# Attention and two MoE layers on one core: where the weight sums of the second layer are made, a second PSUM bank for h, and row moves between ring loads

## The chip, the cores and the metric

The kernel runs on one core of one Trainium2 chip. The metric is the device time of the whole program in microseconds. The kernel before takes 974.08 us (median of three runs, 971.9 to 975.14).

## What is computed

The reference, cut to what matters:

```
def phi(x):                                   # x: (4, 8, 576, 64), omega: (128, 64)
    h = einsum('bhsd,md->bhsm', x, omega) - sum(x * x, -1) / 2
    return exp(h - max(h, -1)) / sqrt(128)
q_p, k_p = phi(q * scale), phi(k * scale)
kv, z = einsum('bhsm,bhsd->bhmd', k_p, v), sum(k_p, axis=2)
attn = (q_p @ kv) / (q_p @ z + 1e-6)          # 4 batches, 8 heads, 576 tokens, 64 wide
x = attn, heads side by side                  # 2304 tokens x 512
h = x @ w_in;   x = (h * clip(h + 3, 0, 6) / 6) @ w_out          # layer 1: 512 -> 2048 -> 512
h = x @ w_in2;  out = (h * sigmoid(1.702 * h)) @ w_out2          # layer 2, same sizes
```

## The kernel before

Every fp32 product is made of three fp32r products of a high part (a rounded copy) and a low part (the value less the copy): high x high, high x low, low x high.

Heads are worked in 16 pairs. Pairs 0 to 4 come first. Pairs 5 to 15 lie inside layer 1. Layer 1 takes the 2304 tokens in chunks of 512, 512, 512, 512 and 256 columns, and each chunk in J = 16 steps n (80 steps). TensorE makes in step n the 12 matmuls of `hidden(n)` into the one PSUM bank `hid`, then the 12 of `output(n - 1)` (6 of 512 columns in the last chunk). Between the two come a unit of an attention pair and behind the second another: each step has two slots g = 2n and 2n + 1, a pair has 8 slots, and its units are in `UNITS` ("q", "tail"; "cross"; "k"; "moves"; none; "kv" with the feature parts; "nd0"; "nd1"). So a new pair begins every fourth step. `hidden(n)` waits on `gated`, until VectorE has read h of step n - 1 out of the bank.

ScalarE makes of h the factor R (`gate`), VectorE multiplies (`gated_block`), ScalarE rounds the product (`high`) and VectorE takes the low part (`low`). In the attention units ScalarE also makes exps, high features (`q_hi`), half of the block moves of q (`moves`, DMAs on its own queue) and the quotient's parts; VectorE makes maxima, biases, the transposes `cross`, the states and low features. GpSimd squares and folds rows of q and k (`square_rows`), which VectorE sums (`norms`) for the biases: the squares of q of pair a + 2 at slot 7 of pair a, those of k of pair a + 1 at slot 2.

Layer 2 is computed by a scheme with 7 products of quarter matrices for 8, for tokens in three parts of 768. It needs sums of quarters of its weights. They are made in 32 half-units u on the way (`load_raw`, `prepare`, `high_combos`, `store_combos`): SP loads 128 x 512 raw weights, GpSimd makes four sums of 128 x 128, ScalarE rounds raw (128 x 384) and sums (128 x 512), GpSimd takes the two low parts, SP stores four pieces (high and low of 384 and 512 columns) to the DRAM tensor `combos`. Of the 32 half-units the first EARLY_PREP = 10 are at every second step from step 14, in one buffer (a free part of X); the others are at steps 49 to 63 and then at every second, in three buffers `stage`. Each engine works through its own list in order, and a wait holds all that stands behind it; SP's list holds, in this order around an early half-unit: the block moves of q (behind `cross`), the stores of half-unit u, the load of u + 1 (which waits until those stores have landed), the columns of the next pair, the stores of u + 1, the load of u + 2, the rows of q, the values and the rows of k.

In layer 2 TensorE takes a unit of 12 matmuls of 384 columns for every 512 KB block that SP loads from `combos` into a ring of 10 slots (`load_combos`). The ring's first 10 loads are put between layer 1's last steps. The last chunk of layer 1 comes out by rows; VectorE transposes it in 32 x 32 blocks (`turned_rows`), and 32 DMAs of 16 KB move the blocks to their places in X (`row_move`). They are needed for the last third of layer 2.

## Time and profile before

| | before |
|---|---|
| median of 3 runs | 974.08 us |
| the profiled execution, its own time | 973.57 us |
| its span | 971.8 us |
| busy: PE, DVE, ACT, POOL | 892.7, 552.6, 428.6, 433.8 us |
| 134 + 34 ring loads, KB each, us to landing | 512.0 KB, 4.4 and 4.3 us |

The span is 1.8 us less than the profiled execution's own time, and that is 0.5 us under the median. PE's busy time has modelled ends, so a stretch of 100% is not a full one; its idle time and the granted clock are the more useful columns. Slots and steps stand in the trace in order: the "q" unit of a pair is the first group of L908 on PE, nd0 is L988.

### The profile page before, as it was taken

The numbers are of one execution on the slowest core, as the hardware profiler recorded it, in microseconds if no ns is written. First come the engines' busy times: TensorE is split into PE (matmuls) and PEld (weight loads), VectorE is DVE, ScalarE is ACT, GpSimd is POOL, SyncE is SP. The second block draws the span as 40 slices with busy tenths as digits, with TensorE's granted clock in tenths as the row PEclk, the third lists the DMA queues.
The fourth block names the chain that finished last, engine by engine and source line by source line (L and its number), as shares of the span: only waits on it lengthen the run. The fifth ranks groups of instructions, "written<-read, shape, count | busy, mean of one in ns | idle before, by whom it ended". The sixth has DMA issues, their size and how long they took to land.

```text
span 971.8 us, 13881 instructions
## 1 busy us (share of the span) xinstructions
PE 892.7 (92%) x5029; PEld 800.7 (82%) x5029; DVE 552.6 (57%) x815; ACT 428.6 (44%) x874; POOL 433.8 (45%) x428
## 2 busy tenths in 40 slices
PE   8999999678596889999999989499899998999998
PEld 8988886567475668888888879399899998999998
DVE  7876677337263566565223346247854478645673
ACT  6866755344343445454344444034343343423432
POOL 3676554334144242002777772267603676036630
PEclk9999999898897979999999999699999999999999
DMA  9546542543625334312777981587688875888882
GB/s 281 161 126 150 150 95 66 165 98 87 152 58 156 85 88 85 62 25 71 208 215 211 310 254 30 181 317 249 198 276 291 253 255 187 277 290 251 255 263 88
DMA packets 186324, 170.54 MB, mean 175 GB/s; under 512 B 87824, under 2 KB 148368, under 8 KB 186256
## 3 DMA queue, kind: packets, MB, share of 16 engines
q1 hardware_dynamic: 164832, 167.00, 57.4%
q10 hardware_dynamic: 21424, 2.65, 1.9%
q8 instruction: 40, 0.66, 0.3%
q14 instruction: 28, 0.23, 0.1%
HBM read 128.52 MB, written 34.08 MB: 167 GB/s over the span
## 4 chain that ended last, share of the span: by engine, by line
PE 66%; DVE 11%; SPq 7%; DMA 6%; POOL 4%; issue 3%; ACT 2%; ACTq 0%; DVEq 0%; POOLq 0%
PE acc L1063 8%; PE acc L1064 8%; PE acc L1065 8%; PE hid L1028 5%; PE hid L1029 5%; PE hid L1006 5%; PE acc L1121 4%; PE acc L1129 4%; PE acc L1128 4%; SPq L604 4%; PE att L1063 2%; PE att L1064 2%; PE att L1065 2%; DVE g L1692 2%; SPq L696 2%
## 5 line engine op out<-in xcount | busy, mean ns | idle before, releaser
L1662 DVE SCALAR_TENSOR_TENSOR R<-R,hid 128x512 f32<-128x512 f32 (+1 forms) x79 | 49.9, 631 | 170.8 <-ACT R L1283 170.8
L827 POOL TENSOR_TENSOR G<-G,gate 128x768 f32<-128x768 f32 x36 | 66.6, 1850 | 138.8 <-ACT gate L1376 138.8
L1028 PE MATMUL hid<-x_hi,w_in_hi 128*128 128x512 f32 (+1 forms) x316 | 123.7, 391 | 5.0 <-DVE R L1662 5.0
L1006 PE MATMUL hid<-x_lo,w_in_hi 128*128 128x512 f32 (+1 forms) x316 | 120.3, 381 | 0.3 <-DVE x_lo L1655 0.3
L1029 PE MATMUL hid<-x_hi,w_in_lo 128*128 128x512 f32 (+1 forms) x316 | 120.0, 380 | 0.0
L1692 DVE TENSOR_TENSOR g<-G,g 128x768 fp32r<-128x768 f32 x72 | 99.8, 1404 | 20.5 <-ACT g L1354 20.4
L1121 PE MATMUL acc<-g_hi,w_out_hi 128*128 128x512 f32 x256 | 101.1, 395 | 1.0 <-DVE g_lo L1667 0.9
L1283 ACT ACTIVATE R<-hid 128x512 f32<-128x512 f32 (+1 forms) x79 | 43.9, 555 | 123.9 <-PE hid L1006 110.0
L1128 PE MATMUL acc<-g_lo,w_out_hi 128*128 128x512 f32 x252 | 98.2, 390 | 0.0
L1129 PE MATMUL acc<-g_hi,w_out_lo 128*128 128x512 f32 x252 | 98.2, 390 | 0.0
L1354 ACT ACTIVATE g<-G 128x768 fp32r<-128x768 f32 x72 | 60.9, 847 | 72.0 <-PE acc L1065 35.4
L1667 DVE TENSOR_TENSOR g_lo<-R,g_hi 128x512 fp32r<-128x512 f32 (+1 forms) x80 | 59.3, 741 | 40.4 <-ACT g_hi L1289 40.3
L1063 PE MATMUL acc<-xhi,ring_hi 128*128 128x384 f32 x192 | 65.1, 339 | 13.9 <-DMA ring_hi<-combos 13.6
L1028 PEld LDWEIGHTS hid<-x_hi,w_in_hi 128*128 128x128 f32 x316 | 62.5, 198 | 18.7 <-DVE R L1662 7.0
L1006 PEld LDWEIGHTS hid<-x_lo,w_in_hi 128*128 128x128 f32 x316 | 62.0, 196 | 12.4 <-DVE x_lo L1655 1.3
L1029 PEld LDWEIGHTS hid<-x_hi,w_in_lo 128*128 128x128 f32 x316 | 62.4, 198 | 9.8
L1063 PE MATMUL acc<-g,ring_hi 128*128 128x384 f32 x192 | 65.3, 340 | 5.3 <-issue 5.3
L1065 PE MATMUL acc<-g,ring_hi 128*128 128x384 f32 x192 | 65.3, 340 | 0.0
L1064 PE MATMUL acc<-g,ring_hi 128*128 128x384 f32 x192 | 65.3, 340 | 0.0
L1376 ACT ACTIVATE gate<-G 128x768 f32<-128x768 f32 x36 | 30.5, 847 | 78.8 <-DVE G L1706 65.1
L1065 PE MATMUL acc<-xlo,ring_hi 128*128 128x384 f32 x192 | 64.9, 338 | 0.0
L1064 PE MATMUL acc<-xhi,ring_hi 128*128 128x384 f32 x192 | 64.9, 338 | 0.0
(270 smaller groups left out, 2235.1 us busy)
## 6 DMA issues: line engine op xcount, KB each, us to landing
ring_hi<-combos SPq DMA_DIRECT2D x134, 512.0 KB, 4.4
ring_lo<-combos SPq DMA_DIRECT2D x34, 512.0 KB, 4.3
combos<-stage SPq DMA_DIRECT2D x44, 256.0 KB, 3.3
combos<-stage SPq DMA_DIRECT2D x44, 192.0 KB, 3.0
stage<-w_raw SPq DMA_DIRECT2D x22, 256.0 KB, 2.9
combos<-X SPq DMA_DIRECT2D x20, 256.0 KB, 3.0
out_t<-X SPq DMA_DIRECT2D x12, 384.0 KB, 5.9
X<-w_in SPq DMA_DIRECT2D x16, 256.0 KB, 3.1
```

Source lines behind the costliest of these rows:

```text
L827: nc.gpsimd.tensor_tensor(g, g, R2[:, k % 2], ALU.mult).then_inc(gated2, 1)
L1006: return nc.tensor.matmul(hid_bank(n)[:, 0:t], w_hi[0][:, s * 512 + k * P:s * 512 + (k + 1) * P], x_lo[:, k, x0:x0 + t], start=False, stop ...
L1028: nc.tensor.matmul(bank, w_hi[0][:, at], x_hi[:, k, x0:x0 + t], start=(k == 0), stop=False)
L1029: nc.tensor.matmul(bank, w_lo[0][:, at], x_hi[:, k, x0:x0 + t], start=False, stop=False)
L1063: nc.tensor.matmul(to, w[:, at:at + P], high[:, k, :], start=opens and k == 0, stop=False, skip_group_check=True)
L1064: nc.tensor.matmul(to, w[:, at + P:at + 2 * P], high[:, k, :], start=False, stop=False, skip_group_check=True)
L1065: last = nc.tensor.matmul(to, w[:, at:at + P], low[:, k, :], start=False, stop=closes and k == 1, skip_group_check=True)
L1121: nc.tensor.matmul(bank, w_hi[1][:, at], g_hi[:, g, 0:t], start=(s == 0), stop=False)
L1128: nc.tensor.matmul(bank, w_hi[1][:, at], g_lo[:, g, 0:t], start=False, stop=False)
L1129: last = nc.tensor.matmul(bank, w_lo[1][:, at], g_hi[:, g, 0:t], start=False, stop=(s == J - 1))
L1354: nc.scalar.activation(g2[q][:, 0], feature(q, p), ACT.Copy).then_inc(g2_high, 1)
L1692: nc.vector.tensor_tensor(g2[q][:, 1], feature(q, p), g2[q][:, 0].bitcast(F32), ALU.subtract).then_inc(g2_ready, 1)
```

## The change

- EARLY_PREP is 8 and not 10. The steps of the first 8 half-units stay. Their rounding goes from ScalarE to GpSimd (`early_combos`, `early_lows`): copy and low part are there on one engine.
- The other 24 half-units: 20 of them at every 8/5 of a half-step in chunk 3 (steps 48 to 63), and 4 at every second step from step 64. They have four buffers, and VectorE, not GpSimd, takes their low parts (`low_combos`). ScalarE and VectorE do theirs between other work of a step (`late_highs`, `late_lows`), three half-steps after the load's place (five for the last four).
- From step TWO_BANKS = 49 odd steps put h into the bank `att2` and R into a buffer `R_odd`. `hidden(n)` then waits for the product of step n - 2, not n - 1, and `gate(n)` on `g_ready` in the same way.
- The 32 row moves no longer stand together ahead of the ring loads from the 11th on: one goes behind each ring load from the 29th to the 60th.
- `x_first_sums(0)`, two sums on GpSimd for layer 2, is made at step 67 and not 75.

```diff
 AFTER = {"u2": 1, "11": 2, "u3": 3, "22": 4, "21": 5, "12": 6}
-EARLY_PREP = 10
+EARLY_PREP = 8
+LAST_PREP = 28
...
     LAST1 = L2 - J
+    TWO_BANKS = 3 * J + 1
     ITEMS = 2 * J
...
         def hid_bank(n):
-            return att[0] if n == 1 else hid
+            return att[0] if n == 1 else att2 if n >= TWO_BANKS and n % 2 else hid
+        def gates_before(n):
+            return n - 1 if n >= TWO_BANKS else n
...
-        def prep_step(u):
-            if u < EARLY_PREP:
-                return 14 + 2 * u
+        def prep_half(u):
             v = u - EARLY_PREP
-            return 49 + v if v < 15 else 64 + 2 * (v - 15)
-        def load_step(u):
-            return prep_step(u) - (1 if u < EARLY_PREP else 2)
-        def preps_at(n, step):
-            return [u for u in range(PREPS) if step(u) == n]
+            return 26 + 4 * u if v < 0 else 6 * J + v * 8 // 5 if u < LAST_PREP else 8 * J + 4 * (u - LAST_PREP)
+        def preps_at(half, early, late_by):
+            return [u for u in range(PREPS) if half == prep_half(u) + (early if u < EARLY_PREP else late_by + 2 * (u >= LAST_PREP and late_by > 2))]
         def stage_of(u):
-            return 3 if u < EARLY_PREP else (u - EARLY_PREP) % 3
+            return (u - EARLY_PREP) % 4 if u >= EARLY_PREP else 4
         def uses_of(u):
-            return u + 1 if u < EARLY_PREP else (u - EARLY_PREP) // 3 + 1
+            return u + 1 if u < EARLY_PREP else (u - EARLY_PREP) // 4 + 1
...
                     weights(j)
+                for u in preps_at(g, 4, 4):
+                    store_combos(u)
+                for u in preps_at(g, 0, 0):
+                    load_raw(u)
                 if g % 2 == 0:
-                    for u in preps_at(g // 2 - 1, prep_step):
-                        store_combos(u)
-                    for u in preps_at(g // 2, load_step):
-                        load_raw(u)
                     for i in range(RING):
                         if g // 2 == LAST1 + ring_frees[i] - 1:
                             load_combos(i)
-            for tile in range(2):
-                sp.wait_ge(rows_turned, tile + 1)
-                for i in range(4):
-                    for j in range(4):
-                        sp.dma_start(*row_move(tile, i, j)).then_inc(rows_moved[tile], 16)
+            row_moves = {A_UNITS + k: (k // 16, k // 4 % 4, k % 4) for k in range(32)}
             stores = {output_unit(c, p, GROUPS2 - 1) + RING: (c, what) for c in range(SUPERS)
                       for p, what in ((3, "11"), (5, "22"), (6, "21"))}
             stores |= {output_unit(c, 6, GROUPS2 - 1) + RING + 2: (c, "12") for c in range(SUPERS)}
             for i in range(RING, SUPERS * UNITS2 + RING + 3):
                 if i < SUPERS * UNITS2:
                     load_combos(i)
+                if i in row_moves:
+                    tile, *of_tile = row_moves[i]
+                    sp.wait_ge(rows_turned, tile + 1)
+                    sp.dma_start(*row_move(tile, *of_tile)).then_inc(rows_moved[tile], 16)
                 if i in stores:
...
                 nc.gpsimd.tensor_tensor(s4, second, s2, ALU.subtract).then_inc(prep_added, 1)
+            def early_combos(u):
+                raw, sums_u, high, sums_high = stage(u)
+                nc.gpsimd.tensor_copy(high, raw[:, 0:3 * P]).then_inc(prep_high, 1)
                 pool.wait_ge(prep_added, 4 * u + 4)
+                nc.gpsimd.tensor_copy(sums_high, sums_u).then_inc(prep_high, 1)
+            def early_lows(u):
+                raw, sums_u, high, sums_high = stage(u)
                 pool.wait_ge(prep_high, 2 * u + 1)
...
                     square_rows(a + 2, KQ)
-                if g % 2 == 0:
-                    for u in preps_at(g // 2, prep_step):
-                        prepare(u)
-                if g == 2 * (LAST1 + 11):
+                for u in preps_at(g, 2, 2):
+                    prepare(u)
+                    if u < EARLY_PREP:
+                        early_combos(u)
+                        early_lows(u)
+                if g == 2 * (LAST1 + 3):
                     x_first_sums(0)
...
                 elif 2 < n:
-                    pe.wait_ge(gated, n)
+                    if n == TWO_BANKS:
+                        pe.wait_ge(den_ready, dens_to(PAIRS - 1, 1, 1))
+                    pe.wait_ge(gated, gates_before(n))
                 bank, x0 = hid_bank(n)[:, 0:t], x_columns(c)[0]
...
                 if 0 < n:
-                    act.wait_ge(g_ready, n)
+                    act.wait_ge(g_ready, gates_before(n))
                 nc.scalar.activation(r, h, ACT.Relu, bias=3.0).then_inc(gate_ready, 1)
...
                 nc.scalar.activation(sums_high, sums_u, ACT.Copy).then_inc(prep_high, 1)
+            def late_highs(half):
+                for u in preps_at(half, 3, 3):
+                    if u >= EARLY_PREP:
+                        high_combos(u)
...
                     next_chunk(n)
+                late_highs(2 * n)
                 if not keys:
                     high(n)
+                late_highs(2 * n + 1)
                 if n == L2 - 1:
...
                         moves(a, 1)
-                for u in preps_at(n, prep_step):
-                    high_combos(u)
                 if n - LAST1 - 12 in (0, 1):
...
                     dve.wait_ge(out_done, (c + 1) * J)
+                    dve.wait_ge(stored_prep[3], 64 * uses_of(PREPS - 1))
                     nc.vector.tensor_scalar(rows_1[:, WIDE:2 * WIDE], acc[1][:], 1.0 / 6.0, None, ALU.mult).then_inc(evac_dve, 2)
...
                     nc.vector.tensor_scalar(x_at(m, token, t), acc[m][:, 0:t], 1.0 / 6.0, None, ALU.mult).then_inc(evac_dve, 1)
+            def low_combos(u):
+                raw, sums_u, high, sums_high = stage(u)
+                dve.wait_ge(prep_high, 2 * u + 1)
+                dve.wait_ge(prep_added, 4 * u + 4)
+                nc.vector.tensor_tensor(raw[:, 0:3 * P].bitcast(F32R), raw[:, 0:3 * P], high.bitcast(F32), ALU.subtract).then_inc(prep_low, 1)
+                dve.wait_ge(prep_high, 2 * u + 2)
+                nc.vector.tensor_tensor(sums_u.bitcast(F32R), sums_u, sums_high.bitcast(F32), ALU.subtract).then_inc(prep_low, 1)
+            def late_lows(half):
+                for u in preps_at(half, 3, 3):
+                    if u >= EARLY_PREP:
+                        low_combos(u)
...
                         attend(a, what)
+                late_lows(2 * n)
                 low(n)
+                late_lows(2 * n + 1)
                 for a, what in now:
```

Three places in the engines' lists. First ScalarE at pair 8, the end of step 16 and what follows, before. X is the raw weights' buffer (384 columns) and the sums' (512); R and g_hi belong to layer 1, q_hi to attention; k_phi, the exps of k, and X<-acc, an evacuation, stand ahead:

```order
L1220 ACTIVATE k_phi<-att,bias 128x128 x8
L1299 ACTIVATE X<-acc 128x512 x2
L1231 DMA q_phi<-q_blocks 32x9x32 x5
L1310 ACTIVATE X<-X 128x384
L1312 ACTIVATE X<-X 128x512
L1283 ACTIVATE R<-hid 128x512
L1236 ACTIVATE q_hi<-q_phi 128x576
```

and in the changed kernel:

```order
L1237 ACTIVATE k_phi<-att,bias 128x128 x8
L1317 ACTIVATE X<-acc 128x512 x2
L1248 DMA q_phi<-q_blocks 32x9x32 x5
L1300 ACTIVATE R<-hid 128x512
L1253 ACTIVATE q_hi<-q_phi 128x576
```

The two rounding copies between the block moves and the factor R are gone from ScalarE; nothing else moved there.

Second GpSimd at the same half-unit, before (squares of rows ahead of it and behind it, four sums, two low parts):

```order
L742 TENSOR_TENSOR rows<-rows 128x9x16
L782 TENSOR_TENSOR X<-X 128x128
L783 TENSOR_TENSOR X<-X 128x128
L785 TENSOR_TENSOR X<-X 128x128
L787 TENSOR_TENSOR X<-X 128x128
L790 TENSOR_TENSOR X<-X 128x384
L792 TENSOR_TENSOR X<-X 128x512
L736 TENSOR_TENSOR rows<-rows 128x576
```

and in the changed kernel:

```order
L747 TENSOR_TENSOR rows<-rows 128x9x16
L787 TENSOR_TENSOR X<-X 128x128
L788 TENSOR_TENSOR X<-X 128x128
L790 TENSOR_TENSOR X<-X 128x128
L792 TENSOR_TENSOR X<-X 128x128
L796 CAST X<-X 128x384
L798 CAST X<-X 128x512
L803 TENSOR_TENSOR X<-X 128x384
L805 TENSOR_TENSOR X<-X 128x512
L741 TENSOR_TENSOR rows<-rows 128x576
```

Two casts stand between the sums and the low parts; the half-unit's place between the squares has not moved.

Third SP at the end of layer 1, before (the last stores, the last two of the first ten ring loads, the row moves of both tiles, and the ring loads from the 11th):

```order
L651 DMA combos<-stage_83 128x3x128
L652 DMA combos<-stage_83 128x4x128
L664 DMA ring_hi<-combos 128x1024 x2
L696 DMA X<-q_cols 32x4x32 x16
L696 DMA X<-k_cols 32x4x32 x16
L664 DMA ring_hi<-combos 128x1024
L664 DMA ring_lo<-combos 128x1024
L664 DMA ring_hi<-combos 128x1024
L664 DMA ring_lo<-combos 128x1024
```

and in the changed kernel, from the seventh of the first ten ring loads to the first row moves:

```order
L669 DMA ring_hi<-combos 128x1024 x5
L669 DMA ring_lo<-combos 128x1024
L669 DMA ring_hi<-combos 128x1024
L669 DMA ring_lo<-combos 128x1024
L669 DMA ring_hi<-combos 128x1024 x7
L669 DMA ring_lo<-combos 128x1024
L669 DMA ring_hi<-combos 128x1024
L669 DMA ring_lo<-combos 128x1024
L669 DMA ring_hi<-combos 128x1024 x5
L707 DMA X<-q_cols 32x4x32
L669 DMA ring_hi<-combos 128x1024
L707 DMA X<-q_cols 32x4x32
```

Ring loads now follow at once on the first ten, and the row moves come one by one behind the 29th and later ones.

## Rows read from the trace of the kernel before

**Rows 1.** Stretches: length; PE, PEld, DVE, ACT, POOL busy; clock; DMA share; GB/s.
```profile
200.00:300.00 100.00, 76.60 (x390) 62.35 (x390) 43.96 (x75) 36.27 (x92) 32.14 (x47) 0.89 0.46 113
480.00:540.00 60.00, 60.00 (x281) 50.25 (x280) 18.24 (x30) 26.51 (x52) 44.78 (x67) 1.00 0.76 220
540.00:590.00 50.00, 45.40 (x271) 40.51 (x270) 19.62 (x32) 22.44 (x47) 30.79 (x40) 0.97 0.82 255
603.00:618.00 15.00, 6.15 (x34) 5.50 (x33) 6.17 (x5) 3.34 (x5) 7.19 (x4) 0.82 0.16 24
```

**Rows 2.** Who waited for whom: us in total, times, longest.
```profile
PE att L988 <- DVE state_lo L1549: 42.3, 5, 9.3
...
ACT X L1310 <- DMA X<-w_raw: 40.1, 5, 8.9
...
PE acc L1063 <- DMA ring_hi<-combos: 13.6, 1, 13.6
```

**Rows 3.** Chain that ended last, in order of time: "q" units of three pairs.
```profile
120.90 1.12 PE att L908 x16
...
354.25 1.09 PE att L908 x16
...
382.77 1.09 PE att L908 x16
```

**Rows 4.** Timeline of ScalarE, pair 8: start, us, instruction, idle before.
```profile
178.10 0.52 ACT L1310 ACTIVATE X<-X 128x384 fp32r<-128x384 f32 x1 [8.00 <-DMA X<-w_raw]
...
180.53 0.58 ACT L1283 ACTIVATE R<-hid 128x512 f32<-128x512 f32 x1
```

**Rows 5.** Timeline of SP's DMA issues, pair 8.
```profile
164.49 5.59 SPq L604 DMA_DIRECT2D q_phi<-q_blocks  x8
...
175.46 0.35 SPq L642 DMA_DIRECT2D X<-w_raw  x1
...
185.30 0.34 SPq L642 DMA_DIRECT2D X<-w_raw  x1
```

**Rows 6.** GpSimd: timeline of pair 8, and the group of its casts.
```profile
178.15 0.46 POOL L782 TENSOR_TENSOR X<-X 128x128 f32<-128x128 f32 x1 [17.59 <-DMA X<-w_raw]
...
188.89 1.15 POOL L736 TENSOR_TENSOR rows<-rows 128x576 f32<-128x576 f32 x1 [6.62 <-DMA rows<-q_n]
...
192.56 0.44 POOL L782 TENSOR_TENSOR X<-X 128x128 f32<-128x128 f32 x1
...
L756 POOL CAST w_out_hi<-X 128x512 fp32r<-128x512 f32 x3 | 1.9, 617 | 0.0
```

**Rows 7.** Timeline of VectorE: end of pair 8, and pair 14 (no half-unit there).
```profile
191.03 1.22 DVE L1667 TENSOR_TENSOR g_lo<-R,g_hi 128x512 fp32r<-128x512 f32 x1 [1.52 <-ACT g_hi L1289]
...
391.49 0.26 DVE L1499 TENSOR_REDUCE half_norm<-rows 128x9 f32<-128x144 f32 x1
...
394.93 0.69 DVE L1662 SCALAR_TENSOR_TENSOR R<-R,hid 128x512 f32<-128x512 f32 x1 [1.51 <-ACT R L1283]
396.31 0.69 DVE L1667 TENSOR_TENSOR g_lo<-R,g_hi 128x512 fp32r<-128x512 f32 x1 [0.70 <-ACT g_hi L1289]
```

**Rows 8.** TensorE: pairs 8 and 14, last chunk, layer 2's 11th and 12th units.
```profile
182.68 0.61 PE L988 MATMUL att<-q_hi,state_hi 128*128 128x288 f32 x1 [8.46 <-DVE state_lo L1549]
...
396.57 0.39 PE L1028 MATMUL hid<-x_hi,w_in_hi 128*128 128x512 f32 x1
...
578.59 0.58 PE L1028 MATMUL hid<-x_hi,w_in_hi 128*128 128x256 f32 x1 [2.67 <-DVE R L1662]
...
624.06 0.66 PE L1063 MATMUL acc<-xhi,ring_hi 128*128 128x384 f32 x1 [13.60 <-DMA ring_hi<-combos]
...
628.03 0.53 PE L1063 MATMUL acc<-xhi,ring_lo 128*128 128x384 f32 x1
```

**Rows 9.** Timeline of SP at the turn to layer 2.
```profile
598.77 10.89 SPq L696 DMA_DIRECT2D X<-q_cols  x16
...
620.00 0.59 SPq L664 DMA_DIRECT2D ring_hi<-combos  x1
```

More of the change, by code:

```diff
@@ L90, in build @@
         g_lo = sb("g_lo", [P, G_SLOTS, CH_MAX], F32R)
+        cols_base = (nc.sbuf_base + 31) // 32 * 32
         xt_a = [sb("q_cols", [P, S + TAIL]), sb("k_cols", [P, S + TAIL])]
@@ L150, in build @@
         g2 = [at_place(f"g2_{i}", [P, 2, 2, HALF2], rows_base + 2 * i * PART, F32R) for i in range(GROUPS2)]
-        late = [at_place(f"stage{i}", [P, 1920], stage_base + i * 1920 * 4) for i in range(3)]
+        late = [at_place(f"stage{i}", [P, 1920], at) for i, at in
+                enumerate([stage_base, stage_base + 7680, stage_base + 15360, cols_base])]
+        R_odd = at_place("R_odd", [P, CH_MAX], cols_base + 7680)
         sum_c = ctx.enter_context(nc.psum_tensor("acc01", [P, 2, 512], F32))
@@ L168, in build @@
         load_w = [sem(f"load_w{i}") for i in range(W_SLOTS)]
-        load_prep = [sem(f"load_prep{i}") for i in range(4)]
-        stored_prep = [sem(f"stored_prep{i}") for i in range(4)]
+        load_prep = [sem(f"load_prep{i}") for i in range(5)]
+        stored_prep = [sem(f"stored_prep{i}") for i in range(5)]
         prep_added = sem("prep_added")
@@ L399, in R_of @@
         def R_of(n):
-            return R[:, 0:size(n)]
+            return (R_odd if n >= TWO_BANKS and n % 2 else R)[:, 0:size(n)]
         def in_rows(c):
@@ L1247, in quotient_part @@
                 if a == PAIRS - PPB and half == 0 and h == 0:
-                    act.wait_ge(stored_prep[3], 64 * EARLY_PREP)
+                    act.wait_ge(stored_prep[4], 64 * EARLY_PREP)
                 nc.scalar.activation(x_at(k, token, HALF, h * D, (h + 1) * D), bank[h * D:(h + 1) * D, 0:HALF], ACT.Copy)
@@ L1294, in evacuate @@
                     act.wait_ge(acc_done, (c + 1) * (KC - 1))
+                    act.wait_ge(stored_prep[3], 64 * uses_of(PREPS - 1))
                     nc.scalar.activation(rows_1[:, 0:WIDE], acc[0][:], ACT.Copy, scale=1.0 / 6.0).then_inc(evac_act, 2)
```

## The prediction

> **What bounds the kernel now.** I read the waits first, then the chain, then the timelines of each engine at the places named there. TensorE is busy nearly all the time in layers 1 and 2, so only its idle time can be won, and it has three kinds. Five times it waits for the states of attention ahead of nd0 (L988), 42.3 us in all [rows 2]. Once it waits 13.6 us for a ring load, at the turn to layer 2 [rows 2]. A few microseconds more are lost in layer 1's last chunk [rows 1]. The name of the releaser at L988 is not the cause. Before one such wait ends, ScalarE has stood 8.00 us in the rounding copy of a raw half-unit (L1310) and comes to R only at 180.53 [rows 4]; VectorE's product, and the states behind it, wait for that R. ScalarE has such a wait five times, 40.1 us [rows 2], as often and about as long as TensorE: the same five places. The load is late because SP works in order: it issues the block moves of q until 170.1, behind them the four stores of the half-unit before, and the load only when these have landed, at 175.46 [rows 5]. It lands at 178.1, when ScalarE and GpSimd start [rows 4, 6]. GpSimd waits for it too, here 17.59 us [rows 6], but that is not yet on the path. At the turn to layer 2 SP issues the row moves from 598.77 on, and the 11th ring load at 620.00 [rows 9]. TensorE has it at 624.06 [rows 8].
>
> How much the five waits cost is read from the pairs. A pair without a half-unit takes 382.77 - 354.25 = 28.52 us [rows 3]. The six pairs from 120.90 to 354.25 take 233.35 us, which is 62.2 more than six times 28.52. The five waits are 42.3 of it. The other 19.9 is matmuls at the lower of the two clock levels after each wait (the granted clock is 0.89 from 200 to 300 us [rows 1]), and small waits where pairs 8 and 12 meet a chunk's border.
>
> **The change, part by part.**
>
> *Rounding of 8 early half-units on GpSimd, two fewer of them.* ScalarE no longer waits for a raw load inside attention. Then R comes when the block moves are issued, at about 170.5. The product takes 0.7 us and the states four short operations; the high features wait until the last moves have landed. I put both at 173.5 at the latest, by the 2.15 us from R to L988 [rows 4, 8] and a landing of 3 us behind 170.1. TensorE asks for them at 182.68 - 8.46 = 174.2 [rows 8]. So I take the wait as gone in all five pairs, and in pair 12 the half-unit itself is gone. Of the 62.2 us I leave 5.0 for the chunk borders, where ScalarE and VectorE still split four blocks: 57.2 us are won, if nothing else is late.
>
> What is late next is GpSimd, and behind it VectorE. A cast of 128 x 512 takes 0.617 us [rows 6]; one of 384 columns 0.5 by its width, so each half-unit holds GpSimd 1.1 us longer. SP's round is: the end of `cross` (164.5) to the load 11.0 us, and 12.3 with the usual ten moves for eight; from this load to the next 185.30 - 175.46 = 9.84, now 10.9; until the rows of q, issued behind it, have come and their squares begin 3.6; the squares 3.7 [rows 5, 6]. So the squares end 30.5 us after the cross of their pair. VectorE sums them right behind the next cross (391.49), which comes 28.5 us after the first: it waits 2.0 us there. It can bear that: it is idle for 1.51 us before its next R, and that R, done at 395.62, is asked for at 396.57 [rows 7, 8], some 2.3 us together. Pair 8 is the exception. It meets a chunk's border. Its "q" unit is at 149.4 (120.90 + 28.52) and its cross ends 15.1 us later, against 8.7 in pair 14 [rows 3, 5, 7]. So the next cross comes after 28.5 - 6.4 and the border's own 3 or so, 25.5 us, and the squares (eight moves there) after 29.2: 3.7 us of waiting, 1.4 beyond the slack. I add 0.5 for each of two further pairs, since a landing there can be a microsecond longer: 2.4 us. The bounds are 0 and 12 us (3 us in each of four pairs, what the whole round is longer if every landing grows as far as the ring loads' 4.4 us). Net: 54.8 us, 45 to 59.
>
> A rule that speaks against this edit: the Trainium skill (GPSIMD Engine Reference, Key points) says that GpSimd shares its SBUF interfaces with VectorE, with contention where VectorE has two SBUF inputs. The trace agrees in kind: a low part of 128 x 512 takes VectorE 0.69 us, and 1.22 us beside GpSimd's squares [rows 7]. By it the added 1.1 us of casts would cost VectorE at most 8 x 0.5 = 4 us, most of it inside its slack; that lies within the bound of 12.
>
> *The 24 late half-units and two banks.* GpSimd's work there falls (four sums are left) and VectorE, 18.2 us busy of 60 [rows 1], gets two low parts, about 1.2 us each half-unit. In steps 48 to 63 TensorE shows no wait, so nothing can be won there. In the last chunk (540 to 590) it is idle 50.0 - 45.4 = 4.6 us [rows 1], the longest wait 2.67 [rows 8], and the clock of 0.97 is at least 1.5 us more in matmuls at the lower level: 6 to 7 us. There 4 half-units stand for 7, the two sums of X are out of the way, and the second bank lets R be one step later. But ring loads and half-units still share SP and the DMA engines, and copies wait in line on two engines now. I take 4.5 us won; bounds 6.8 won and 10 lost. The loss would be in chunk 3: a half-unit moves 0.26 MB in and 0.92 MB out, 1.18 MB; at 220 GB/s it takes 5.4 us [rows 1], one step. Five half-units in four steps need 275 GB/s, a DMA share of 0.76 x 275 / 220 = 0.95. There four buffers and about three half-steps of lead cover a few microseconds of lateness.
>
> *Row moves between ring loads.* The 11th ring load is issued when the first unit is done, long before 610. TensorE's 13.60 us go, and with them the slow matmuls after it: the 11th unit takes 3.97 us [rows 8] where 12 matmuls of 384 columns need 2.0 (281 of 512 columns in 60 us [rows 1], three quarters of it for each), and the slow stretch goes on into the next unit, 2.8 us in all. I take 16.0 us, leaving 0.4 for a new wait on VectorE or ScalarE, which used the pause to catch up; bounds 13 and 16.5. The moves' own cost: from 603 to 618 some 22 of them keep the DMA engines 0.16 busy, 2.4 us, so 0.11 us each [rows 1, 9]. SP has 2.0 us per unit for a load and a move, some 0.6 us each.
>
> The Trainium skill (DMA: Bandwidth & Descriptors, Specifications) asks for at least 512 B a transfer for line rate, and the row moves have pieces of 128 B. By it they could slow the ring loads beside them; by the share of 0.16 all 32 take 3.5 us of DMA time in 32 units, which the ring's lead of nine units covers.
>
> *Sum.* 54.8 + 4.5 + 16.0 = 75.3 us. The profiled execution's own time is 973.57 us (span 971.8), which gives 898.3; the median is 0.5 us higher, so 898 to 899. I say 898.
>
> **The rivals.**
> 1. *GpSimd's and SP's round becomes the bound in attention.* For it: the round is 28 us long against a pair of 28.5, so nothing is to spare, and every store is waited for before the next load. Against it: only four pairs have half-units. Each of them 3 to 6 us longer (matmuls at the lower clock included) gives 12 to 24 us less: 910 to 922.
> 2. *The late stretch turns into waits.* At a DMA share of 0.95 ScalarE and VectorE both stop for raw loads and stores; 5 to 15 us are lost there in place of 4.5 won: 908 to 918.
> 3. *Slower than before.* The same mechanism at full size, in chunk 3: 20 half-units in line on ScalarE and VectorE. To eat the 75 us each would have to take 4.35 + 3.8 = 8.1 us, so a buffer's whole round 32 us with four buffers. Its parts here are a load of 2.6 us, four sums of 0.46, 5.4 for the stores and their landing [rows 5, 6], and at most a step of waiting for its place. Only a load that stood behind ring loads each time would come near. Then 980.
> 4. *The change doesn't do what it says:* the early waits have another cause than L1310 (q's block moves), and TensorE waits at L988 as before. Then only the turn and the last chunk are won: 953.
>
> **How the numbers follow.** Forecast as told, 892 to 905: 0.50. Rival 1: 0.25. Rival 2: 0.17. Rival 4: 0.04. Rival 3: 0.03. The rest, 0.01, is nothing moved. The range 889 to 920 holds the forecast's own range, most of rivals 1 and 2 and the most that can be won (59 + 7 + 16.5 = 82.5 us, 891). A measurement of this kernel tells about 0.3% from no change. Faster 0.96, same 0.01, slower 0.03.
>
> **What would show it.** Right: no wait of ScalarE for w_raw in attention; TensorE waits at L988 for 5 us in all at most; "q" units of pairs 8 to 13 about 29 us apart; GpSimd still waits for early raw loads, and VectorE now waits for squares (L1499 of before) once for some 4 us; no wait for a ring load at the turn, with the first units 2.1 us each; DMA share over 0.9 in chunk 3 with TensorE idle for under 3 us. Wrong: pairs of 32 us and more with VectorE waiting for GpSimd's squares (rival 1); ScalarE waiting for `stage` loads and TensorE for g_lo in chunk 3 (rival 2); L988 still waiting 8 us (rival 4).

## The result, and the profile after

The changed kernel takes 903.25 us (median of four runs, 902.23 to 905.13), against 974.61 us for the kernel before in the same series (four runs). The ratio is 0.9275, 95% interval 0.9249 to 0.9300: 71.4 us won where 75.3 were forecast. The profiled execution took 905.13 us, the slowest of the four; its span is 903.3 us against 971.8, so 68.5 us are to be found between the two traces.

**Attention.** "q" units of pairs 8, 10, 13 and 14, from the chain of the changed kernel (compare [rows 3]; L908 is now L923):

```profile
149.76 1.12 PE att L923 x16
...
212.49 1.12 PE att L923 x16
...
303.00 1.09 PE att L923 x16
...
331.51 1.09 PE att L923 x16
```

Pairs 8 to 12 take 303.0 - 149.8 = 153.2 us, and 204.8 before (from TensorE's timeline): 51.6 us won. One by one they are 32.6, 30.1, 28.7, 30.2 and 31.6 us long, where a pair alone takes 28.5. The stretch that was [rows 1]'s first now has TensorE busy for 96.8 us of 100 at a granted clock of 1.00 (the higher level throughout). Stretches of the changed kernel (columns as in rows 1):

```profile
200.00:300.00 100.00, 96.83 (x543) 79.53 (x542) 70.43 (x115) 49.81 (x126) 52.24 (x71) 1.00 0.57 143
424.00:454.00 30.00, 30.00 (x134) 24.86 (x133) 17.76 (x26) 13.54 (x26) 16.82 (x32) 1.00 0.87 259
454.00:480.00 26.00, 26.00 (x117) 21.52 (x116) 12.65 (x22) 11.02 (x23) 12.27 (x25) 1.00 0.93 280
480.00:512.00 32.00, 27.37 (x159) 24.05 (x158) 20.53 (x35) 13.51 (x32) 13.81 (x22) 0.95 0.94 288
```

The waits, for those of [rows 2]:

```profile
POOL X L787 <- DMA X<-w_raw: 29.0, 4, 15.6
...
DVE half_norm L1522 <- POOL rows L747: 8.0, 3, 3.7
```

ScalarE has no wait for a raw load and TensorE none at nd0 (now L1003). GpSimd still waits for the loads, and nothing in attention waits for the half-units' sums. What is new is VectorE's wait for GpSimd's squares. Pair 9 shows where it comes from. SP (for [rows 5]):

```profile
175.74 0.35 SPq L647 DMA_DIRECT2D X<-w_raw  x1
...
187.74 0.35 SPq L647 DMA_DIRECT2D X<-w_raw  x1
188.12 0.43 SPq L586 DMA_DIRECT2D rows<-q_n  x1
```

GpSimd at the same half-unit (for [rows 6]), then VectorE ([rows 7]) and TensorE ([rows 8]) behind the squares:

```profile
180.85 0.61 POOL L798 CAST X<-X 128x512 fp32r<-128x512 f32 x1
181.43 1.02 POOL L803 TENSOR_TENSOR X<-X 128x384 fp32r<-128x384 f32 x1
182.40 1.71 POOL L805 TENSOR_TENSOR X<-X 128x512 fp32r<-128x512 f32 x1
191.32 1.15 POOL L741 TENSOR_TENSOR rows<-rows 128x576 f32<-128x576 f32 x1 [7.20 <-DMA rows<-q_n]
...
194.19 0.50 POOL L747 TENSOR_TENSOR rows<-rows 128x144 f32<-128x144 f32 x1
```

```profile
194.72 0.31 DVE L1522 TENSOR_REDUCE half_norm<-rows 128x9 f32<-128x144 f32 x1 [3.60 <-POOL rows L747]
```

```profile
174.27 0.29 PE L1003 MATMUL att<-q_hi,state_hi 128*128 128x288 f32 x1
...
197.60 0.50 PE L1045 MATMUL hid<-x_hi,w_in_hi 128*128 128x512 f32 x1 [1.25 <-DVE R L1685]
```

At 174.27, where TensorE stood for 8.46 us before, there is no wait. But the load of the next half-unit now comes 12.0 us after this one's (9.84 before), the rows of q stand behind it on SP, their squares end at 194.69, VectorE waits 3.60 us for them, makes the biases and R after that, and TensorE waits 1.25 us for R.

**The late stretch.** From pair 14's "q" unit to the first unit of layer 2 it takes 534.1 - 331.4 = 202.7 us, and 585.86 - 382.70 = 203.2 before: half a microsecond won. In chunk 3 the DMA share is 0.93 and TensorE is not idle at all. In the last chunk (480 to 512) it is idle for 4.6 us. That is as much as before, but not the same waits: the four of before (0.52, 0.72 and 2.67 us for R, 0.68 us for g_lo) are gone, and three others have come:

```profile
483.81 0.50 PE L1138 MATMUL acc<-g_hi,w_out_hi 128*128 128x512 f32 x1 [1.34 <-DVE g_lo L1690]
488.62 0.47 PE L1055 MATMUL acc<-w_out_hi,g_hi 128*128 128x512 f32 x1 [0.36 <-DVE X L1704]
505.85 0.80 PE L1055 MATMUL acc<-w_out_hi,g_hi 128*128 128x512 f32 x1 [2.92 <-DVE g_lo L1690]
506.45 0.63 PE L1056 MATMUL acc<-w_out_hi,g_lo 128*128 128x512 f32 x1
```

The longest ends on a low part of layer 1 that VectorE was late with. VectorE and GpSimd just before it:

```profile
493.43 0.56 DVE L1710 TENSOR_TENSOR stage<-stage 128x384 fp32r<-128x384 f32 x1
493.95 0.69 DVE L1712 TENSOR_TENSOR stage<-stage 128x512 fp32r<-128x512 f32 x1
...
500.04 2.11 DVE L1710 TENSOR_TENSOR stage<-stage 128x384 fp32r<-128x384 f32 x1 [0.96 <-POOL stage L792]
502.07 2.30 DVE L1712 TENSOR_TENSOR stage<-stage 128x512 fp32r<-128x512 f32 x1
```

```profile
499.90 1.84 POOL L821 TENSOR_TENSOR x_sum<-X 128x768 f32<-128x768 f32 x1
501.82 2.01 POOL L823 TENSOR_TENSOR X<-X 128x768 f32<-128x768 f32 x1
503.79 0.90 POOL L787 TENSOR_TENSOR stage<-stage 128x128 f32<-128x128 f32 x1
```

The same two low parts take 1.25 us at 493 and 4.41 us at 500, where GpSimd makes its two sums of X (the changed `x_first_sums(0)`): 3.16 us more, and behind them TensorE waits 2.92 us and then works at the lower clock (0.63 us for a matmul of 0.40; the granted clock is 0.81 from 503 to 512 us), which costs 0.19 x 9, some 1.7 us.

In the kernel before, GpSimd made the two sums at step 75, and they met VectorE there too, at a low part of layer 1:

```profile
569.27 1.84 POOL L808 TENSOR_TENSOR x_sum<-X 128x768 f32<-128x768 f32 x1
```

```profile
569.31 2.09 DVE L1667 TENSOR_TENSOR g_lo<-R,g_hi 128x256 fp32r<-128x256 f32 x1 [0.48 <-ACT g_hi L1289]
```

TensorE waited 0.68 us for that g_lo. In the changed kernel two instructions of VectorE in a row stand beside the two sums, and R and g_lo of layer 1 stand behind both.

**The turn.** SP's first ring loads behind those of layer 1's end, and TensorE's first two units (for [rows 9] and [rows 8]):

```profile
532.92 3.83 SPq L669 DMA_DIRECT2D ring_hi<-combos  x2
538.52 0.32 SPq L669 DMA_DIRECT2D ring_lo<-combos  x1
```

```profile
534.14 0.33 PE L1080 MATMUL att<-xhi,ring_hi 128*128 128x384 f32 x1
...
536.25 0.33 PE L1080 MATMUL acc<-xhi,ring_lo 128*128 128x384 f32 x1
```

No wait for a ring load is left. The first 20 units take 45.3 us (534.14 to 579.40), and 61.7 before (585.86 to 647.60): 16.5 won. The rest of layer 2 is the same to 0.3 us. Sum: 51.6 + 0.5 + 16.5 = 68.6 of 68.5 us.

### The profile page after: what moved, and what is told of

Same layout as the page of the kernel before. It is cut to its first block, busy times and chain, and to the rows that moved or that the text cites. A ratio compares the mean times of both kernels' runs of the same rounds, so it can differ in the third digit from the quotient of the medians.

```text
span 903.3 us, 13874 instructions
## 1 busy us (share of the span) xinstructions
PE 878.0 (97%) x5029; PEld 789.7 (87%) x5029; DVE 590.2 (65%) x863; ACT 418.5 (46%) x858; POOL 396.6 (44%) x396
## 4 chain that ended last, share of the span: by engine, by line
PE 74%; DVE 10%; DMA 4%; POOL 3%; issue 3%; SPq 3%; ACT 2%; ACTq 0%; DVEq 0%; POOLq 0%
PE acc L1080 9%; PE acc L1082 8%; PE acc L1081 8%; PE acc L1138 5%; PE acc L1146 4%; PE acc L1145 4%; PE hid L1045 4%; PE hid L1021 4%; PE hid L1046 4%; PE att L1080 3%; PE att L1082 3%; PE att L1081 3%; PE att L960 2%; DVE g L1729 2%; PE att L923 2%
## 5 line engine op out<-in xcount | busy, mean ns | idle before, releaser
L1045 PE MATMUL hid<-x_hi,w_in_hi 128*128 128x512 f32 (+1 forms) x252 | 98.0, 389 | 2.8 <-DVE R L1685 2.8
L1021 PE MATMUL hid<-x_lo,w_in_hi 128*128 128x512 f32 (+1 forms) x252 | 95.6, 379 | 0.9 <-DVE x_lo L1678 0.7
L1046 PE MATMUL hid<-x_hi,w_in_lo 128*128 128x512 f32 (+1 forms) x252 | 94.9, 377 | 0.0
L1300 ACT ACTIVATE R<-hid 128x512 f32<-128x512 f32 (+1 forms) x63 | 36.0, 572 | 94.7 <-PE hid L1021 77.9
L1685 DVE SCALAR_TENSOR_TENSOR R<-R,hid 128x512 f32<-128x512 f32 (+1 forms) x63 | 40.9, 649 | 57.7 <-ACT R L1300 57.6
L787 POOL TENSOR_TENSOR stage<-stage 128x128 f32<-128x128 f32 x24 | 14.9, 621 | 121.6 <-DMA stage<-w_raw 121.6
L1690 DVE TENSOR_TENSOR g_lo<-R,g_hi 128x512 fp32r<-128x512 f32 (+1 forms) x64 | 48.1, 752 | 27.0 <-ACT g_hi L1306 26.8
L1658 DVE RECIPROCAL k_phi<-k_phi 128x288 f32<-128x288 f32 x24 | 46.8, 1949 | 20.6 <-ACT k_phi L1267 20.6
L1138 PEld LDWEIGHTS acc<-g_hi,w_out_hi 128*128 128x128 f32 x256 | 48.1, 188 | 13.9 <-DVE g_lo L1690 3.1
L1045 PEld LDWEIGHTS hid<-x_hi,w_in_hi 128*128 128x128 f32 x252 | 47.5, 188 | 13.6 <-DVE R L1685 3.8
```

Source lines behind the costliest of these rows:

```text
L1021: return nc.tensor.matmul(hid_bank(n)[:, 0:t], w_hi[0][:, s * 512 + k * P:s * 512 + (k + 1) * P], x_lo[:, k, x0:x0 + t], start=False, stop ...
L1045: nc.tensor.matmul(bank, w_hi[0][:, at], x_hi[:, k, x0:x0 + t], start=(k == 0), stop=False)
L1046: nc.tensor.matmul(bank, w_lo[0][:, at], x_hi[:, k, x0:x0 + t], start=False, stop=False)
L1138: nc.tensor.matmul(bank, w_hi[1][:, at], g_hi[:, g, 0:t], start=(s == 0), stop=False)
```

## The experiments

The kernel before was run anew beside each series (973.02, 975.67 and 971.81 us in the three). The changed kernel was not. The runs of one kernel lie within 0.2 to 0.6% of each other, and the medians of the kernel before in different series up to 3.9 us apart, so a difference of 4 us and less between a run and the changed kernel's 903.25 is not shown by the medians; for those I give the stretches of the traces, and the waits in them.

**Rounding on GpSimd alone** (all ten early half-units, everything else as before):

```diff
+                if u < EARLY_PREP:
+                    nc.gpsimd.tensor_copy(high, raw[:, 0:3 * P]).then_inc(prep_high, 1)
+                    pool.wait_ge(prep_added, 4 * u + 4)
+                    nc.gpsimd.tensor_copy(sums_high, sums_u).then_inc(prep_high, 1)
...
                 for u in preps_at(n, prep_step):
-                    high_combos(u)
+                    if u >= EARLY_PREP:
+                        high_combos(u)
```

> The kernel before, with the rounding of all 10 early half-units on GpSimd and nothing else. My theory: ScalarE's wait for the raw load was the cause of the five waits ahead of nd0, and this one edit is worth about 50 us (the changed kernel's pairs 8 to 12 take 153.2 us for 204.8), so 974.6 - 50 = 923 to 927; pair 12 keeps a half-unit here and may be 1 to 2 us longer. Rival (the load itself, or the block moves behind it, is what TensorE waits for): the waits at nd0 stay at 8 us each and the time within 5 us of 974.

Measured: 932.52 us, ratio 0.9588 (0.9562 to 0.9615), 40.5 us less and not 50. The four pairs 8 to 11 are 32.7, 30.1, 28.8 and 29.5 us long, within 0.1 us (pair 11: 0.7) of the changed kernel's, so this edit alone is the cause there. Pair 12 is 43.4 us long (41.0 in the kernel before), which I had not expected. Its ScalarE and TensorE rows:

```profile
306.74 0.40 ACT L1253 ACTIVATE X<-att 64x288 f32<-64x288 f32 x1 [11.11 <-DMA combos<-X]
```

```profile
307.62 0.61 PE L992 MATMUL att<-q_hi,state_hi 128*128 128x288 f32 x1 [7.59 <-ACT k_phi L1254]
```

The quotient of pair 12 writes to the part of X that is the early half-units' buffer, so it waits until the stores of the tenth have landed (SP issues the last of them at 303.7 us), 11 us too late. The wait for the states ahead of nd0 is gone in this pair too, but of the gain in pair 12 the rounding gives nothing: it comes from "8 for 10".

**Row moves alone** (the changed kernel's edit at the ring, in the kernel before):

> The kernel before, with the row moves one by one behind the 29th to 60th ring load and nothing else. My theory: 16.5 us less (13.6 of waiting and 2.8 of slow matmuls), 958; no wait for a ring load is left. Rival (128 B pieces beside the ring loads slow them): a wait for ring loads of some microseconds appears in units 20 to 50, and the time is 960 to 965.

Measured: 957.17 us, ratio 0.9831 (0.9792 to 0.9869), span 955.1. SP at the turn:

```profile
597.79 14.94 SPq L664 DMA_DIRECT2D ring_hi<-combos  x7
614.49 0.32 SPq L664 DMA_DIRECT2D ring_lo<-combos  x1
...
629.41 0.60 SPq L702 DMA_DIRECT2D X<-q_cols  x1
```

The ring loads go on through the stretch that the 32 moves had taken, the first 20 units take 45.2 us, 16.5 less, and no wait for the ring is left, in units 20 to 50 either: the moves of 128 B pieces between the loads hold up nothing that TensorE waits for. This term stands by itself.

**Ten half-units and not eight, in the changed kernel** (the waits that name the last half-units' stores follow suit):

```diff
-EARLY_PREP = 8
-LAST_PREP = 28
+EARLY_PREP = 10
+LAST_PREP = 30
```

> The changed kernel with 10 early half-units again (22 late ones, the last 2 at every second step). With the early rounding alone ScalarE stood 11.1 us in pair 12 for the landed stores of half-unit 9, because the quotient of pair 12 writes where the early buffer lies. If that wait is what the 8 for 10 took away, this kernel has a pair 12 of 43 us for 31.5 and is 11 us slower than the changed one, 914. Rival (the late stretch with fewer half-units gives back as much): under 908.

Measured: 916.47 us (915.56 to 917.14), ratio 0.9402 (0.9380 to 0.9425), 13 us more than the changed kernel by the medians and 10.1 by the spans. Pairs 8 to 12 take 12.9 us more, nearly all of it in pair 12 with 44.1 us, and the late stretch 1.9 less. The waits are those of the first experiment:

```profile
ACT X L1266 <- DMA combos<-X: 11.0, 1, 11.0
...
PE att L1003 <- ACT k_phi L1267: 7.5, 1, 7.5
```

By the spans, rounding alone (41.6 us less than before), row moves alone (16.7) and "8 for 10" (10.1) add up to 68.4 of the 68.5 us.

**GpSimd's sums of X back at step 75:**

```diff
-                if g == 2 * (LAST1 + 3):
+                if g == 2 * (LAST1 + 11):
                     x_first_sums(0)
```

> The changed kernel with the two sums of X on GpSimd at step 75 again, not 67. My theory: at step 67 they run beside VectorE's two low parts of a half-unit, which take 2.11 and 2.30 us there for 0.56 and 0.69 elsewhere, and TensorE waits 2.9 us for R and g_lo and has about 2 us of slow matmuls after it. Then this kernel is 4 to 5 us faster than the changed one, 898 to 899, with low parts of 0.6 and 0.7 us. Rival (the low parts are slow because their sums or stores come late, whatever GpSimd does): the same 903, with the long operations still at step 68.

Measured: 904.7 us, ratio 0.9295 (0.9269 to 0.9321): nothing won. My expectation took the program's step for the time. GpSimd is not tied to TensorE's steps: it comes to the sums as soon as its last half-unit ahead of them is done, and meets VectorE's low parts of just this half-unit, one later than in the changed kernel. The low parts at 500 us are no longer the slow ones; those at 512 us are:

```profile
511.85 1.85 POOL L821 TENSOR_TENSOR x_sum<-X 128x768 f32<-128x768 f32 x1
513.77 2.04 POOL L823 TENSOR_TENSOR X<-X 128x768 f32<-128x768 f32 x1
```

```profile
512.00 2.11 DVE L1710 TENSOR_TENSOR stage<-stage 128x384 fp32r<-128x384 f32 x1 [0.97 <-POOL stage L792]
514.03 2.33 DVE L1712 TENSOR_TENSOR stage<-stage 128x512 fp32r<-128x512 f32 x1
```

**GpSimd's sums held until the low parts are taken.** Now the place on GpSimd is as in the changed kernel, and a wait parts the two:

```diff
                 if g == 2 * (LAST1 + 3):
+                    pool.wait_ge(prep_low, 2 * (LAST_PREP + 1) + 2)
                     x_first_sums(0)
```

> The changed kernel with a wait on GpSimd: the two sums of X start when VectorE's low parts of the half-unit before them are done. Moving them to step 75 did not part them, since GpSimd runs ahead of TensorE and came to them right behind the last half-unit's sums, again beside two low parts (2.11 and 2.33 us). With contention as the cause, no low part is over 0.8 us now, the wait for g_lo at 505.9 us (2.9 us and slow matmuls after it) goes, and the time falls by 4 us, to 899. Rival (low parts are slow for another reason): a low part over 2 us is still there, and 903.

Measured: 899.22 us (898.34 to 900.75), ratio 0.9228 (0.9205 to 0.9250), 4.0 us less than the changed kernel. The low parts are short again, and the sums take as long as ever:

```profile
497.42 0.55 DVE L1711 TENSOR_TENSOR stage<-stage 128x384 fp32r<-128x384 f32 x1
497.92 0.69 DVE L1713 TENSOR_TENSOR stage<-stage 128x512 fp32r<-128x512 f32 x1
```

```profile
498.69 1.85 POOL L821 TENSOR_TENSOR x_sum<-X 128x768 f32<-128x768 f32 x1 [1.47 <-DVE stage L1713]
500.62 1.91 POOL L823 TENSOR_TENSOR X<-X 128x768 f32<-128x768 f32 x1
```

Of TensorE's 2.92 us wait 0.45 is left, and from pair 14 to layer 2 it is 199.0 us, not 202.7. One of layer 1's low parts, at 499.61 us, still takes 1.21 us beside the first sum, so the meeting is smaller and not gone. It is the meeting of the two engines that costs, not either engine's amount of work. It comes with VectorE's new low parts, and not with the sums' move from step 75 to 67: put back there, they meet the next ones.

**One bank for h:**

```diff
-    TWO_BANKS = 3 * J + 1
+    TWO_BANKS = 10 * J + 1
```

> The changed kernel with one PSUM bank for h and one R throughout. If the second bank hides the half-units' work on ScalarE and VectorE, this loses 5 to 10 us: 908 to 913, with TensorE waiting for R in chunk 3, where a half-unit's copies (1.1 us) and low parts (1.25 us) fall into the 2.7 us between h and the next h. Rival (the chain from h to g_lo is the tighter one, and it has a whole step either way): within 2 us of 903.

Measured: 903.54 us, ratio 0.9284 (0.9259 to 0.9309), the time of the changed kernel. In chunk 3 TensorE waits for nothing with one bank either. In the last chunk the waits are 4.3 us in all (4.6 with two banks), the longest now ahead of `hidden` and not of `output`, since with one bank it is the product R that TensorE lacks first:

```profile
483.42 0.50 PE L1138 MATMUL acc<-g_hi,w_out_hi 128*128 128x512 f32 x1 [1.34 <-DVE g_lo L1690]
...
503.42 0.39 PE L1045 MATMUL hid<-x_hi,w_in_hi 128*128 128x256 f32 x1 [2.31 <-DVE R L1685]
```

The second bank is worth nothing that can be measured. The rival's reading holds.

**Layer 1's own copies always ahead of the half-unit's** on ScalarE and VectorE:

```diff
-                late_lows(2 * n)
                 low(n)
+                late_lows(2 * n)
                 late_lows(2 * n + 1)
```

(and `late_highs` in the same way behind `high`).

> The changed kernel with each step's rounding copies and low parts of half-units always behind high and low of layer 1, never ahead of them. The wait for g_lo of 1.34 us at 483.8 us, where step 63 has a half-unit's copies and low parts between the chunk's split and g_lo, should go, and with it some of the 0.4 at 488.6: 1.5 us less, which the profile shows better than the times. Rival (the split alone makes g_lo late there): the same wait of 1.3 us.

Measured: 901.97 us (901.08 to 904.26), ratio 0.9263 (0.9238 to 0.9287). The wait at the chunk's border moves rather than goes, from 1.34 us at 483.81 to

```profile
488.48 0.57 PE L1055 MATMUL acc<-w_out_hi,g_hi 128*128 128x512 f32 x1 [1.96 <-DVE X L1704]
```

where it ends on an evacuation. So the wait that I expected to go did not. The times cannot tell the 1.3 us won from noise; the trace has the late stretch 1.7 us shorter, at the step where the slowed low parts stood (0.86 us of waiting in place of 2.92): g_lo is now ahead of them.

**Rows of q ahead of the next half-unit's stores** on SP:

```diff
-                a = at_slot(g, 6)
+                a = at_slot(g, 4)
                 if a is not None and a + 2 < PAIRS:
                     rows_of(a + 2, KQ)
+                a = at_slot(g, 6)
                 if a is not None and a + 1 < PAIRS:
                     values(a + 1)
```

> The changed kernel with SP's load of the rows of q of pair a + 2 two slots earlier, ahead of the stores and the load of the second half-unit of a pair. My theory: the waits for R at 197.6 and 256.5 us (1.25 and 1.35 us) come from VectorE's wait for GpSimd's squares of these rows, so they go and the time falls by 2.5 to 3 us, with pairs 9 and 11 at 28.6 us for 30.1 and 30.2. Rival (VectorE is late there for its work beside GpSimd, not for the squares): nothing changes. A cost that I can't exclude: GpSimd's squares now come ahead of a raw load's landing and the second half-unit's stores come later by what the rows' load takes, some 0.5 us.

Measured: 899.48 us (896.94 to 901.62), ratio 0.9228 (0.9202 to 0.9253), 3.8 us less. The pairs are 31.0, 28.5, 28.6, 29.3 and 30.6 us long, 147.9 us in all and not 153.2: 5.3 us, more than I expected, since the border pairs 8 and 12 gain 1.6 and 1.0 too. VectorE waits for these squares no more. TensorE's wait for R at pair 9 (1.25 us) is gone; of the 1.35 us at pair 11, 0.43 is left. In the other kernels with eight early half-units and the old order pairs 8 to 12 take 151.9 to 153.9 us, in the three with the new order 147.4 to 147.9.

**Both edits**, this one and the held sums:

> The changed kernel with two of the edits tried so far together: the rows of q are loaded ahead of the next half-unit's stores (alone 3.8 us less than the changed kernel), and GpSimd's two sums of X wait until VectorE has taken the low parts of the last late half-unit of chunk 3 (alone 4.0 us less). If the two costs are what I say, squares that come late in attention and VectorE's low parts slowed by GpSimd's sums in the last chunk, they lie 250 us apart, on different waits, and add up: 7.8 to 9.5 us less than the changed kernel, 894 to 895.5 us. The rival is that both edits win by the same thing (for instance by the place of something behind them, or by a chance offset of the late stretch); then together they win 4 to 5 us, 898.5 to 899.5.

Measured: 896.11 us (895.19 to 897.01), ratio 0.9219 (0.9194 to 0.9243) beside a kernel before that was 2.8 us faster in this series; 7.1 us less than the changed kernel by the medians, 5.5 by the ratios, 9.0 by the spans (894.3 us; the changed kernel's profiled execution was a slow one by 1.9). These lie on both sides of the gap between the two expectations, so the stretches must decide: attention's five pairs take 147.8 us (5.4 less than in the changed kernel) and the late stretch 198.8 us (3.9 less), each about what its edit won alone, with the same waits gone. The two costs are apart and add up. With the next one this is the fastest kernel of the study, 0.8% under the changed one.

**All three edits:**

> As the kernel with both edits, and ScalarE and VectorE take the high and low parts of late half-units always behind layer 1's own copy and low part of the step, never between. Alone this won 1.3 us, most of it at the step where VectorE's low parts met GpSimd's sums, which the other edits have already cleared. So I expect no more than 0.7 us beside the kernel with both, 893.5 to 895.5 us. If it is 1.3 us or more below that one, the wait at the chunk's border (1.34 us before the first output product of step 63) was worth its full length after all.

Measured: 896.16 us (894.29 to 897.76), ratio 0.9217 (0.9190 to 0.9244): no difference. The wait at the border is again not gone but moved (1.96 us at 483.30), and was not worth its length.

**The late stretch in all twelve kernels.** Lengths from pair 14's "q" unit to layer 2, TensorE's idle time in them, and the granted clock of their last 54 us:

| kernel | us | idle | clock |
|---|---|---|---|
| before | 203.2 | 4.6 | 0.97 |
| rounding on GpSimd alone | 203.0 | 4.5 | 0.97 |
| row moves alone | 203.0 | 5.3 | 1.00 |
| changed | 202.7 | 4.6 | 0.97 |
| sums of X at step 75 | 203.1 | 4.5 | 0.97 |
| one bank | 201.3 | 4.3 | 1.00 |
| ten half-units | 200.8 | 4.0 | 1.00 |
| rows of q first | 201.6 | 4.9 | 1.00 |
| layer 1's own first | 201.1 | 2.8 | 0.97 |
| sums held | 199.0 | 2.2 | 1.00 |
| both | 198.8 | 2.0 | 1.00 |
| all three | 200.3 | 2.3 | 0.97 |

Less the idle time, and less 0.03 x 54 = 1.6 us where the clock is 0.97, all are 196.4 to 197.7 us long. So the lower clock is a term of its own. With rows of q first TensorE waits 3.19 us at the meeting and the matmuls behind it are at the higher level; in the changed kernel it waits 2.92 and they are at the lower one for some 1.7 us. Of the 3.7 us that the held sums win against the changed kernel's trace 2.5 are waiting, and the rest is this clock, which a kernel with the meeting need not pay. Each row is one execution.

## Why the prediction was right, and where it was off

The time lies within the range and the likeliest case was the one that came. Between the two traces, though, 68.6 us were won for 75.3 forecast: two of the three terms were too high, by 3.2 and 4.0 us. The median, 71.4 us won, hides a part of that, since the profiled execution was the slowest of four. By the steps of the prediction:

- **The cause of the five waits** (ScalarE's copy L1310, not the states that the wait is put down to): right. With the rounding moved alone TensorE's wait for the states is gone in all five pairs, and four of them are as short as in the changed kernel.
- **Pair 12:** the number was right and its reason was not the whole one. I put it down to "the half-unit itself is gone". What the two runs with ten half-units show is a second wait that stands behind the first: the quotient's, for stores of the last half-unit, 11 us long. I had not looked for who else uses the buffer.
- **Attention, 54.8 us:** 51.6 measured. The places of the loss are those that I named. VectorE's wait for the squares is 3.60 us at pair 9, where 3.7 was worked out. That is partly luck: the squares end 30.0 us after the cross of pair 8 and not 29.2, and VectorE is ready for them after 26.4 and not 25.5 (28.5 - 6.4 + 3 is 25.1, too), and the two misses cancel. There were two more waits, for which I had put 0.5 us of TensorE's time each: 0.69 at pair 10, and at pair 11 one as long as the first, 3.69, which cost TensorE 1.35. The step that was short is SP's round: 12.0 us from load to load, not 10.9, since the low part of 512 columns took GpSimd 1.71 us and not 1.27 (the casts took 0.51 and 0.61, as worked out), and the stores behind it came later still. The 1.71 us is contention in the other direction: VectorE had started its g_lo at 181.74, and held it until 182.99. Over the chunk borders, pairs 8 and 12 lose 4.1 and 3.0 us, 7.1 and not 5.0; the other three lose 3.5 and not 2.4. The experiment with the rows of q first shows that part of the border's loss too was SP's order.
- **Late half-units and two banks, 4.5 us:** 0.5 measured, the term that failed. Rival 2 did not come: at a DMA share of 0.93 TensorE waits for nothing in chunk 3. The last chunk's old waits went, as forecast, and as much came back. I credited the second bank, which is worth nothing that can be measured, and "the two sums of X out of the way", which they are not: GpSimd comes to them beside VectorE's new low parts, at step 67 as at step 75. This meeting costs 2.5 us of waiting and, in the changed kernel's trace, some 1.2 of the lower clock; without it the term would have been some 4.2. I had priced VectorE's new work by its own length, 1.2 us a half-unit, and not by what it could meet. What the four buffers and the new places of the half-units give by themselves no run shows.
- **Row moves, 16.0 us:** 16.5 measured in both kernels that have the edit.

**How large the contention is.** I had taken 0.5 us for each meeting. Its size follows from the rows. A low part on VectorE that starts inside a two-input sum of GpSimd ends shortly after that sum: the one at 500.04 would wait until 501.74 and then need its 0.56, 2.26 us in all, and takes 2.11; the next would by the same reading take 1.76 + 0.69 = 2.45 and takes 2.30. The 1.22 us of [rows 7] is the same thing. GpSimd at that place in the kernel before:

```profile
190.89 0.81 POOL L740 TENSOR_TENSOR rows<-rows 128x288 f32<-128x288 f32 x1
191.78 0.82 POOL L742 TENSOR_TENSOR rows<-rows 128x144 f32<-128x144 f32 x1
```

VectorE starts at 191.03, the sum ends at 191.70, 0.67 + 0.69 = 1.36, and it takes 1.22; GpSimd's next, 0.50 us alone, in turn takes 0.82. So the price of such a meeting is not a share of the work but up to the whole length of the other engine's instruction, and I should have read it from the longest of them, 1.85 us. The Trainium skill (SBUF — State Buffer, "SBUF: two separate sides") states this, for a VectorE instruction with two inputs in SBUF against one of GpSimd that reads SBUF: the pair of ports is locked for a whole instruction by whichever starts first, and the other stands. The trace agrees, with 0.14 to 0.15 us less than a full stand in all three cases.

## What to carry to other kernels

When work leaves one engine's queue, look at what else hangs on the same buffer and on the same issuing queue: here one wait hid a second of the same length, and a load that stood behind stores set the squares. When work goes to VectorE, look at which of GpSimd's long two-input instructions can meet it, and part them with a wait and not with a step number, because an engine that runs ahead makes its work when its inputs are there. A second buffer is worth only what its wait costs in the trace, less the wait that stands behind it; here the 2.31 us that TensorE waits for R with one bank were 2.92 for g_lo with two. And before a gain of some microseconds is put down to an edit, see whether the granted clock of the stretch is the same in both traces.

## What the runs showed of the hardware

Two-input instructions of VectorE beside two-input instructions of GpSimd over 768 columns took 2.11 and 2.30 us in place of 0.56 and 0.69, three to four times as long, while GpSimd's own went from 1.85 and 1.91 us to 1.84 and 2.01. Where VectorE had started first, GpSimd's low part of 128 x 512 took 1.71 us in place of 1.27. The DMA engines held a share of 0.93 at 280 GB/s for 26 us, with loads and stores in one queue, and TensorE waited for nothing. After waits of 2 to 3 us in the last chunk TensorE's matmuls were at the lower clock level in some kernels and not in others (2.92 us in the changed kernel, yes; 3.19 us with the rows of q first, no).
